# One run of 48 attention tiles with windowed keys, value means on GpSimd, and batch 0's token mixing between batch 1's tiles

## The reference, cut to what matters

```python
k_sum = k.reshape(B, H, nb, 32, D).max(axis=3)      # 24 block maxima of the keys
v_sum = v.reshape(B, H, nb, 32, D).mean(axis=3)     # 24 block means of the values
scores_l = where(|i - j| < 16, q @ k.T / 8, -1e9)   # 768 x 768, a narrow band
scores_s = q @ k_sum.T / 8 + log(32)                # 768 x 24
a = exp(scores - max); a = a / (sum(a) + 1e-9)
x = a @ concat([v, v_sum])                          # (B, 768, 512) once heads are joined
u = x + (relu(x.T @ w_tok1) @ w_tok2).T             # token mixing
y = u + relu(u @ w_ch1) @ w_ch2                     # w_ch1: 512 x 1536
z = y + relu(layernorm(y) * g @ w2_ch1) @ w2_ch2    # w2_ch1: 512 x 2048
```

## Time and profile before

| | us |
|---|---|
| median of 3 executions | 650.66 (650.54 to 652.85) |
| the profiled execution: its span, first to last instruction | 642.7 |
| median less that span: what lies around the instructions | 8.0 |
| first `weigh` of batch 0 | 16.28 |
| batch 0's last tile done | 63.9 |
| first `weigh` of batch 1 | 85.7 |
| batch 1's last tile done | 137.95 |
| first matmuls of the channel layers | 155.9 |
| end | 642.7 |

### The profile page before, as it was taken

One profiled execution on the slowest core, in us unless ns is written; L12 is line 12 of the kernel. 1 busy time (PEld: TensorE's weight loads), 2 busy tenths in 40 slices (PEclk: granted clock), 3 DMA queues, 4 the chain that ended last, 5 costly groups with the idle time before them and its releaser, 6 DMA issues.

```text
span 642.7 us, 9475 instructions
## 1 busy us (share of the span) xinstructions
PE 615.6 (96%) x3232; PEld 538.1 (84%) x3232; DVE 232.6 (36%) x593; ACT 173.6 (27%) x386; POOL 29.0 (5%) x66
## 2 busy tenths in 40 slices
PE   6989988899999999999999999999999999999997
PEld 3767766678998998899899899989998899989996
DVE  5577446655533211311554552123211421131111
ACT  3667237652421111110243331021111111121110
POOL 2123022210000000000000000000000000000000
PEclk9989989999999999999999999999999999999999
DMA  8665145630530000000033210001000100010001
GB/s 203 168 165 143 40 102 142 159 106 1 163 99 1 2 0 1 1 0 0 0 99 122 74 34 2 0 1 50 0 1 0 50 0 0 0 49 1 0 1 49
DMA packets 42650, 32.62 MB, mean 51 GB/s; under 512 B 7308, under 2 KB 35832, under 8 KB 42616
## 3 DMA queue, kind: packets, MB, share of 16 engines
q1 hardware_dynamic: 41920, 31.63, 17.3%
q10 hardware_dynamic: 696, 0.56, 0.3%
HBM read 28.44 MB, written 3.15 MB: 49 GB/s over the span
## 4 chain that ended last, share of the span: by engine, by line
PE 90%; DMA 5%; issue 2%; DVE 1%; ACT 1%; SPq 1%; DVEq 0%; POOL 0%; ACTq 0%; PEldq 0%; POOLq 0%
PE bank L357 87%; DMA v_own<-v 4%; PE bank L492 1%; DMA k_sb<-k_t 1%; PE bank L395 1%; PE bank L396 0%; PE bank L397 0%; DMA v_far<-v_mean 0%; ACT probs L571 0%; DVE natural L797 0%; ACT probs_t L579 0%; SPq L237 0%; DVE natural L871 0%; DVE k_sb L690 0%; SPq L263 0%
## 5 line engine op out<-in xcount | busy, mean ns | idle before, releaser
L847 DVE SCALAR_TENSOR_TENSOR hidden<-bank,hidden 128x384 fp32r<-128x384 f32 x112 | 62.5, 558 | 315.7 <-ACT hidden L610 315.6
L610 ACT ACTIVATE hidden<-bank 128x384 fp32r<-128x384 f32 x112 | 55.0, 491 | 360.6 <-PE bank L357 360.6
L357 PE MATMUL bank<-in_t,slots_low 128*128 128x384 f32 x768 | 144.1, 338 | 2.0 <-issue 1.7
L357 PE MATMUL bank<-slots_low,hidden 128*128 128x512 f32 x576 | 144.1, 395 | 0.0
L357 PEld LDWEIGHTS bank<-in_t,slots_low 128*128 128x128 f32 x768 | 135.4, 188 | 8.2 <-issue 2.9
L357 PEld LDWEIGHTS bank<-slots_low,hidden 128*128 128x128 f32 x576 | 107.5, 188 | 19.7
L357 PE MATMUL bank<-in_t,slots_high 128*128 128x384 f32 x576 | 107.1, 336 | 2.1 <-issue 2.1
L357 PE MATMUL bank<-slots_high,hidden 128*128 128x512 f32 x432 | 108.1, 395 | 0.0
L357 PEld LDWEIGHTS bank<-in_t,slots_high 128*128 128x128 f32 x576 | 101.2, 188 | 6.9 <-issue 3.7
L357 PEld LDWEIGHTS bank<-slots_high,hidden 128*128 128x128 f32 x432 | 79.7, 188 | 14.5
L357 PE MATMUL bank<-k_sb,q_sb 128*128 128x364 f32 x96 | 41.2, 514 | 2.8 <-POOL k_sb L346 2.8
(11 more groups left out here) (67 smaller groups left out, 378.0 us busy)
## 6 DMA issues: line engine op xcount, KB each, us to landing
stage<-w_ch SPq DMA_DIRECT2D x56, 256.0 KB, 3.0
k_sb<-k_t SPq DMA_DIRECT2D x16, 192.0 KB, 4.8
q_sb<-q_t SPq DMA_DIRECT2D x8, 384.0 KB, 5.7
v_own<-v SPq DMA_DIRECT2D x8, 384.0 KB, 6.3
tok_stage<-w_tok SPq DMA_DIRECT2D x8, 384.0 KB, 3.4
out<-natural SPq DMA_DIRECT2D x12, 256.0 KB, 2.1
v_far<-v SPq DMA_DIRECT2D x32, 18.8 KB, 4.8
v_far<-v_mean SPq DMA_DIRECT2D x16, 36.6 KB
```

The costliest lines, as they stand in the source:

```text
L357: return nc.tensor.matmul(dst, lhs, rhs, start=start, stop=stop, skip_group_check=True)
L610: nc.scalar.activation(hidden[:, f % HID_RING, 0, :], ch1_bank[f % 2][:, 0:GN], ACT.Relu).then_inc(hid_high, 1)
L847: nc.vector.scalar_tensor_tensor(out=hidden[:, f % HID_RING, 1, :], in0=ch1_bank[f % 2][:, 0:GN], scalar=0.0, in1=hidden[:, f % HID_RING, ...
```

## The change

- **One run.** The loop over batches goes; tiles 0 to 47 are written out in one sequence, pairs r = 0 to 7, without a restart between the batches.
- **Keys in windows.** The host lays out, for each tile, 128 + 30 keys side by side, overlapping those of the next tile, and leaves 24 columns for the block maxima. The load brings them in one piece per head; POOL's neighbour copies go. Three buffers (`KB = 3`) for keys and queries. The first key load waits for all clears (`k_clear`).
- **Values.** `v_own` arrives as the host laid it out, with its columns of ones; two loads bring the neighbours (`v_edge`). A third copy of the values, transposed (`v_turned`), is loaded for the means.
- **Means.** POOL adds 32 values by a tree of five instructions (16, 8, 4, 2, 1 per block; `sum_values`), TensorE transposes the sums inside `turn` of a pair's tile 2 (`turn_sums`), ACT scales and copies them.
- **Mixing of batch 0.** Its 72 matmuls are spread over tiles 25 to 42, after `weigh`: 3 with each of the first 12, 6 with each of the last 6. Batch 1's mixing comes after the tiles, with hidden matmuls for its first rows ahead of the last tile.
- **Splits.** POOL splits x (both parts) except for the last two; DVE does the low part of the token weights, once instead of twice. Four weight chunks are split during the tiles, four between the tiles and the channel layers, the others in the first group, two in each of its 12 steps.
- **Weights** are laid out by the host in the order in which they are loaded.

The core of the diff:

```diff
+            def load_k(r):
+                i = r % KB
+                if r >= KB:
+                    sp.wait_ge(qk_done, NT * (r - KB + 1))
+                else:
+                    sp.wait_ge(k_clear, CLEARS)
+                for h in range(2):
+                    sp.dma_start(k_sb[64 * h:64 * h + 64, i, :, h * NK:(h + 1) * NK],
+                                 k_w[r // PAIRS, r % PAIRS, 64 * h:64 * h + 64]).then_inc(ld_k[i], 16)
...
+            def load_v(r):
+                i, b, p = r % 2, r // PAIRS, r % PAIRS
+                if r >= 2:
+                    sp.wait_ge(vsum_done, r - 1)
+                sp.dma_start(v_turned[:, i, :], v_t[b, p]).then_inc(ld_vt[i], 16)
+                if r >= 2:
+                    sp.wait_ge(pv_done, NT * (r - 1))
+                else:
+                    sp.wait_ge(far_init, r + 1)
+                sp.dma_start(v_own[:, i], v_w[b, p]).then_inc(ld_v[i], 16)
...
+            def spread_keys(r):
+                i = r % KB
+                for h in range(2):
+                    at = SUM_AT[h]
+                    ks = k_sb[64 * h:64 * h + 64, i]
+                    pool.wait_ge(kmax_done, 2 * r + h + 1)
+                    nc.gpsimd.tensor_copy(ks[:, 1:NT, at:at + NSUM],
...
+                                          ).then_inc(k_ready, 1)
+
+            def sum_values(r):
+                pool.wait_ge(ld_vt[r % 2], 16 * (r // 2 + 1))
+                pool.wait_ge(k_ready, 2 * r + 2)
+                src, lo = v_turned[:, r % 2, :].rearrange("p (n s) -> p n s", s=BLOCK), 0
+                for j, n in enumerate(TREE):
+                    last = n == 1
...
+                    op = nc.gpsimd.tensor_tensor(dst, src[:, :, 0:n], src[:, :, n:2 * n], ALU.add)
+                    if last:
+                        op.then_inc(vsum_done, 1)
+                    else:
+                        op.then_inc(tree_step, 1)
+                        pool.wait_ge(tree_step, 4 * r + j + 1)
+                        src, lo = v_tree[:, :, lo:lo + n], lo + n
...
-            def value_means(b, p, warm_up=False):
...
+            def turn_sums(r, dst):
+                pe.wait_ge(vsum_done, r + 1)
+                nc.tensor.transpose(dst, v_sum[:, r * NSUM:r * NSUM + P], ident[:]).then_inc(mean_done, 1)
...
+            def turn(n):
+                r, t = divmod(n, NT)
+                pe.wait_ge(exp_done, 2 * n + 2)
...
+                if t == MEANS_AT and r + 1 < NPAIR:
+                    turn_sums(r + 1, tb[:, mean_at])
+                nc.tensor.transpose(tb[:, 0:P], pr[:, 0:P], ident[:])
...
+            for n in range(-1, NTILE):
+                if n + AHEAD < NTILE:
+                    mask_scores(n + AHEAD)
...
+                r, t = divmod(n, NT)
+                if n % GT == GT - 1:
+                    normalise(n // GT)
+                if t in (0, 1) and r + 1 < NPAIR:
+                    key_maxima(r + 1, t)
+                if r < TOK_CH and t == 4:
+                    tok_low_part(r)
+                if n == MIX0 + NT - 1:
+                    low_h(0, 0, mix_bank)
...
```

More of the change, by code:

```diff
@@ new lines, in send_means @@
+            def send_means(r):
+                i = r % 2
+                sp.wait_ge(mean_copied, r + 1)
+                if r >= 2:
+                    sp.wait_ge(pv_done, NT * (r - 1))
+                for h in range(2):
+                    at = SUM_ROW[h]
+                    sp.dma_start(v_far[at:at + NSUM, i, :, 1 + h * D:1 + (h + 1) * D],
+                                 v_mean[:, i, h * D:(h + 1) * D].rearrange("p (t n) -> p t n", t=1)
+                                 .broadcast_to([NSUM, NT, D])).then_inc(ld_mean[i], 16)
@@ L242, in load_v @@
[L242 to L299, removed]
@@ new lines, in _ @@
+            load_q(1)
+            load_v(1)
+            send_means(0)
+            load_k(2)
+            load_q(2)
+            for r in range(NPAIR):
+                if r < TOK_CH:
+                    load_tok(r)
+                if r >= TOK_CH:
+                    load_first(r - TOK_CH)
+                if r + 1 < NPAIR:
+                    send_means(r + 1)
+                if r + KB < NPAIR:
+                    load_k(r + KB)
+                    load_q(r + KB)
+                if r + 2 < NPAIR:
+                    load_v(r + 2)
@@ L448, in start, with mix_hidden, mix_out @@
-            def start(b, warm_up=False):
-                scores(b, 0)
-                value_means(b, 0, warm_up)
-                scores(b, 1)
+            def mix_hidden(b, m, t, dst):
+                at = (t % 3) * TOK + m * P
+                last = three(dst[:], lambda s: tok_w[:, s, t // 3, at:at + P],
+                             lambda s: x_split[:, b, s, t, :], t == 0, t == NT - 1)
+                if t == NT - 1:
+                    last.then_inc(tok1_done, 1)
+            def mix_out(t, m, dst):
+                last = three(dst[:], lambda s: tok_w[:, s, 2 + m, t * P:(t + 1) * P],
+                             lambda s: h_tok[:, s, m, :], m == 0, m == 1)
+                if m == 1:
+                    last.then_inc(tok2_done, 1)
@@ L461, in turn_first @@
                     last.then_inc(in_turned, 1)
-            pe.sem_inc(qk_done, QK0)
-            pe.sem_inc(pv_done, PV0)
             pe.wait_ge(warm_ready, 1)
             for _ in range(WARM):
-                mm(mean_bank[:], warm[:, 0:P], warm[:], True, True)
-            pe.wait_ge(k_clear, 4 * K_CLEARS)
-            start(0, warm_up=True)
-            pe.wait_ge(ld_ident, 16)
-            with pe.Fori(0, B) as b:
-                n_all = PAIRS * NT
-                for n in range(-1, n_all):
-                    if n + AHEAD < n_all:
-                        scores(b, n + AHEAD)
-                    if 0 <= n + 1 < n_all:
-                        turn(b, n + 1)
-                    if n >= 0:
-                        weigh(b, n)
-                        if n % NT == MEANS_AT and n // NT + 1 < PAIRS:
-                            value_means(b, n // NT + 1)
-                mix_tokens(b)
+                mm(mix_bank[:], warm[:, 0:P], warm[:], True, True)
@@ new lines, in _ @@
+            pe.wait_ge(k_clear, CLEARS)
+            scores(0)
+            scores(1)
+            scores(2)
+            pe.wait_ge(ld_ident, 16)
+            pe.wait_ge(init_done, 3)
+            turn_sums(0, mix_bank[:, mean_at])
+            turn(0)
+            for n in range(NTILE):
[5 more added lines that the diff above has]
+                mix_first_batch(n)
+                if n == NTILE - 2:
+                    pe.wait_ge(x_low_end, 1)
+                    pe.wait_ge(x_low, 2 * NPAIR - 2)
+                    for t in range(GT):
+                        mix_hidden(1, 0, t, score_bank[1])
@@ L670, in _ @@
+            high_x(2 * NPAIR - 1)
+            for m in range(2):
+                high_h(1, m, score_bank[1 - m])
+            inputs_high(0, 0, (0, 1))
+            for w in range(KEPT, KEPT + 2):
+                split(w)
             inputs_high(0, 0, (2, 3))
+            for w in range(KEPT + 2, 2 * KEPT):
+                split(w)
             group(0, 0, first=True)
@@ L737, in inputs_low @@
                     ).then_inc(in_low, 1)
-            def start(b):
-                for n in range(2):
-                    mask_scores(b, n)
-            dve.sem_inc(u_done, USED0)
-            dve.sem_inc(tok_split, 1)
-            dve.sem_inc(w_split, STAGES)
-            nc.vector.memset(v_own[:, :, :, 0:PV:PV - 1], 1.0).then_inc(init_done, 1)
-            for i in range(2):
-                nc.vector.memset(turn_bank[i][96:P, P:2 * P], 0.0).then_inc(init_done, 1)
-            for i in range(2):
-                clear_keys(nc.vector, 0, i)
```

608 lines of the change are left out of this document (308 added, 300 removed).

## The result

The changed kernel takes 681.53 us (median of 4, 680.61 to 683.85) against 651.65 (4 executions, 650.54 to 652.85) for the kernel before: a ratio of 1.048, with a 95% interval of 1.0436 to 1.0524. It is slower by about 30 us. The forecast was 684.8, with a range of 665 to 699.

A forecast was written before the change was run, and what follows sets the result against it. TensorE was taken as the bound, busy 615.6 of 642.7 us; the front part, with seven waits of 6.3 + 1.7 us, ends at 190.6 against 156.5, +34.1, so span 676.8, plus 8.0 makes 684.8 us; range 665 to 699.

The forecast's parts named there:

- first `weigh`: Start of the tiles: first weigh moves from 16.28 to 20.5 us, bounds 18.5 and 23.
- the seven gaps: TensorE before the transposes of the sums, once a pair, r = 0 to 6: 6.3 us idle each.
- low clock behind a gap: TensorE's restart after each of the seven gaps: 1.7 us lost at the low clock, bounds 0 and 2.5.
- channel layers start: End of the front part: all four input columns ready at 190.6 us, where 156.5 compares before.
- span: Whole profiled execution: 642.7 us plus 34.1 gives 676.8.
- time less span: Median time over profiled span: 8.0 us, taken from the kernel before, 650.66 against 642.7.
- The wait: `turn_sums` in TensorE's queue waits for mask, key maxima, spread and sums behind `scores(6r + 4)`: 6.3 us, seven times.
- The rival on GpSimd's speed: Sums on GpSimd: short runs cost half as much again, 690 us, or with 0.3 overhead per level, 701; 14 in 100.
- That the clock might stay high: TensorE behind the seven gaps: no fall of the clock, 673 us; 15 in 100.
- the forecast's chain: Scores to sums: spread ends 20.21, sums 3.3, signal 0.12, so TensorE goes on at 23.63, not 17.36: 6.3 us.
- the 0.4 that the forecast gave to the hidden layer: Iterations 30 and 36: DVE takes out the hidden layer ahead of `mask_scores`, 0.4 us each, 0.8 in all.
- The rival with no gap: Wait for the sums hidden because they come early enough: 684.8 - 56.8 = 628 us; 7 in 100.

The follow-up runs named there:

- four filled gaps: Changed kernel with 24 bfloat16 matmuls into an unused bank in front of the wait, in the first four of seven gaps: 671.3 us.
- the run with gaps of about 2 us: Changed kernel with the sums transposed in tile 4 of a pair, not tile 2: 641.1 us, ratio 0.990 to the kernel before.
- b1_early: Changed kernel with sums of pair r + 1 between the two splits of x and their load first in SP's round: 624.83 us, ratio 0.962.
- b4_tok_at_2: Changed kernel with the split of the token weights in tile 2 of a pair, not tile 4: 675.07 us.
- the two repeats: On one chip, the changed kernel as it is, 681.26 us, and with the token split in tile 2, 675.49 us.
- the kernels without gaps: Changed kernel with sums between the splits of x and early load, 624.83 us; also without SP's wait for clears, 622.77, or with token split in tile 2, 625.76.

## Why the prediction was right

Forecast and result by its own steps:

| step | forecast | measured |
|---|---|---|
| first `weigh` | 20.5 | 20.2 |
| the seven gaps | 7 x 6.3 = 44.1 | 42.7 (5.42 to 6.63), errors cancel in part |
| low clock behind a gap | 1.7 | 2.5 (10 us for four; 1.9 or 3.2 each) |
| channel layers start | 190.6 | 193.1 |
| span | 676.8 | 679.1 |
| time less span | 8.0 | 2.2 |
| time | 684.8 | 681.5 |

- **The wait** was the whole matter, and it came as read from the order in the queues. The edits show it from four sides: shorten the sums, let TensorE come later, take the sums out of the chain, take them out of every wait. The rival on GpSimd's speed falls, at both of its prices: two-input additions on short runs cost what the long one had promised, 1.00 us for 384 elements and 0.24 for 24. The Trainium skill's half as much again for a strided read (GPSIMD Engine Reference, Performance pitfalls for Q7 kernels) is for steps of more than 8 bytes. Only the last addition, 24 elements, reads so, which by that figure would add about 0.03 us (an estimate: half of 2.1 ns for each); the forecast's rival put it on all 744. No run here shows it.
- **The clock** was mis-sized. The term took one restart of the kernel before, where a tile and a half were slow. After the longer gaps the clock is at 1.2 GHz from before the restart to some 4 us behind it in three cases and some 6 in the other four, and four filled gaps give back 2.5 us each. Seven times the missing 0.8 are 5.6 us, the largest error in the sum of the front part. The Trainium skill's rule (TensorE: Matmul & The Clock Gate, HAM oscillation), that a wait in every round starts every round at the low clock, holds in this trace: in all seven restarts of the changed kernel the transpose of `v_sum` takes 0.45 us, where 0.27 is usual. That the clock might stay high is refuted for gaps over 5 us; in the run with gaps of about 2 us it was so behind three of six.
- **The gap's size** came out right in part by luck. Counted as the trace counts it, from the end of the `scores` matmul (17.00 + 0.83), the forecast's chain gives 5.8 us and not 6.3, and its sums were 0.45 too long: that leaves the 5.42 of the first gap. The next four are 0.9 to 1.2 longer by a term left out: DVE is late at the mask of tile 6r + 4 (2.3 us behind its `scores` matmul and not 1.1), behind the token split. With the split in tile 2 these four are 5.42 too, though `normalise` stays where it was. Moving it saved 5.8 us in all, 3.9 of them in the gaps. The forecast took DVE's part from a tile early in the run, where the split was not in the way. The last two gaps, 5.86 us, have the 0.4 that the forecast gave to the hidden layer.
- **The rival with no gap** was priced at 628 from the forecast's pieces; the kernel that has none takes 624.8.
- **The offset** of 8.0 us between time and span was wrong. Every execution with both numbers has 1.8 to 2.2. By that, the profiled execution of the kernel before took about 644.7 us (an estimate), under all four beside it: it was one of its fastest. In 7 executions beside `b1_early` its time ran from 644.5 to 653.6 and its span from 642.6 to 651.7. The front part was forecast 2.5 us too short and the offset 5.8 too long; the two errors partly cancel in the time. That the time came within 3.3 us is in so far luck.

## What to carry to other kernels

Before a wait is put into an in-order queue, list what must be done for it, in each engine's program order, from the last thing that the waiting engine itself does for that chain. If that is the instruction just before the wait, the whole chain is idle time, however idle the engines in it are. Look at each engine's backlog at that place too: 1 us of split on DVE, three tiles earlier, made four gaps longer. And a shift of the wait by two tiles can be worth more than the rest of the change: 40 us here for one constant, 57 for the right place in two queues. And price an edit in the kernel that it goes into: the same one gave 6 us here and cost 3 there.

## What the runs showed of the hardware

- The granted clock is at its low level behind every gap of 5.4 us or more (seven of seven here, and in the three more profiles with such gaps, `b4_tok_at_2` and the two repeats); behind gaps of 2.06 us it was low twice and high once, so the length alone does not tell. bfloat16 matmuls into an unused bank during the gap held it at 2.4 GHz three times. At the first gap it was already low before them; it rose while they ran, and they took 6.11 us and not 5.35.
- The kernel before varies by 1.4% from execution to execution (7 of them) and the kernels without gaps by 0.3 to 0.5% (4 each). In its seven executions beside `b1_early` the mean granted clock by and large goes with the span: 0.997 at 642.6 us, 0.992 at 644.6 and 646.2, 0.984 at 648.5, 0.987 at 649.0, 0.982 at 650.6, 0.984 at 651.7. Its gaps of 2.4 to 3.1 us are of the length behind which the clock sometimes fell; that this is the cause was not tried.
- A two-input GpSimd addition takes 0.24 us for 24 elements and 1.00 for 384, with 0.08 us to the next one that waits for it, where 0.19 was assumed.
